# Column norms of q and k from one broadcast product, in a fused attention and two-layer kernel on one core

## The chip, the core and the metric

One core of a Trainium2 chip runs the whole program. TensorE (PE) multiplies matrices and loads its weights ahead of them (PEld), VectorE (DVE) and ScalarE (ACT) work on tiles in SBUF and PSUM, GpSimd (POOL) and SyncE (SP) mostly issue transfers. Each engine runs its own instructions in their order, and semaphores join them. The metric is the time of one execution on the device, in microseconds; less is better. The times are medians of several runs.

## What is computed

The inputs q, k and v are 6016 x 256. Each column of q and k is divided by its norm, and the softmax runs over the 256 columns of q for each column of k:

```python
qn = q / (np.linalg.norm(q, axis=1, keepdims=True) + 1e-06)
kn = k / (np.linalg.norm(k, axis=1, keepdims=True) + 1e-06)
s = kn.transpose(0, 2, 1) @ qn / tau
s = s - s.max(-1, keepdims=True)
a = np.exp(s)
a /= a.sum(-1, keepdims=True) + 1e-09
x = v @ a                                   # 6016 x 256
h = x @ w_in                                # 256 -> 2048
x2 = (s1 * np.maximum(h, 0) ** 2 + b) @ w_out
h2 = x2 @ w_in2
out = (np.maximum(h2, 0) + alpha * np.minimum(h2, 0)) @ w_out2
```

## The kernel before

The kernel never forms v @ a. It folds the 256 x 256 matrix a into the first layer's weights (a @ w_in, eight blocks w1_block) and then treats both layers alike: 12 runs (6 pairs of token tiles for each layer) of 8 steps, each step with seven 512-column products on x and four on g, and each product in three passes over halves hi and lo of its operands. That main part starts near 56 us and goes to the end.

The change lies ahead of it, from about 40 to 56 us. Until 40 us the rows of q and k come in by 16 chunks (CHUNKS). ScalarE squares them into sq, VectorE adds the squares into sq_sum, and TensorE builds k^T q (scores, into s_acc) chunk by chunk. It does so in two halves, m = 0 and m = 1, of 128 columns of k each (the partitions of s_acc). For the last six chunks (late onward) the second half is put off, so that the first half is whole early. Then comes a chain over four engines:

- TensorE sums the squares over the partitions into cols_ps, a column of four numbers for each partition: 128 columns of q twice, 128 of k twice.
- ScalarE takes the root. VectorE refines it with one Newton step (reciprocal, times the sum, plus the root, halved, plus 1e-6) and inverts it, four columns wide (rnorm).
- The norms of q are needed along the free dimension. So VectorE writes them on a diagonal (rq_diag), TensorE multiplies that with ones, and ScalarE copies the product out (rq_row).
- For each half m: largest(m) on VectorE makes the logits, their maximum and its negative. soften(m) on ScalarE takes Exp and its sum. turn_a(m) on TensorE transposes, and a_copy(m) on ScalarE copies that half of a to SBUF. inverse_sum(m) on VectorE gives the scale for w1_copy.

Between these, in fixed places, stands the preparation of the first two token tiles. turn_v(0, t, b) turns a square-blocked tile of v on VectorE (two instructions for each t). x_high(0, i) on ScalarE writes the hi half of operand i, x_low(0, i) on VectorE the lo half, and x_sums makes the four sums of tiles. The operands come in the order X_ORDER: i = 0 and 1 are the first tile's blocks and need two turns, i = 2 is a block of the second tile and needs all four:

```python
sc.wait_ge(v_turned, 2 * CB * run + (2, 2, 4)[min(i, 2)])
```

w1_block(0) and (1) need the first half of a, w1_block(2) and (3) the second (a_copied); behind them TensorE starts step 0. The order on each engine is written out by hand. link(...) makes VectorE wait for its own instruction before the next one.

Of the kernel before, what the change touches and what calls it, by code (L numbers as in the profile page):

```python
# [5 lines left out]
ACT = mybir.ActivationFunctionType  # L6
ALU = mybir.AluOpType
# [79 lines left out]
def build(nc, q, k, v, tau, moe_w_in, moe_w_out, moe_s, moe_b, moe2_w_in, moe2_w_out, moe2_alpha, out):  # L87
# [17 lines left out]
    with ExitStack() as ctx:  # L105
# [49 lines left out]
        rq_row = at("rq_row", 170 * K, [C], F32)  # L155
        rq_diag = at("rq_diag", 171 * K, [CB, P], F32)
# [3 lines left out]
        root = col[:, 4:8]  # L160
        rroot = col[:, 8:12]
        ratio = col[:, 12:16]
        twice = col[:, 16:20]
        norm = col[:, 20:24]
        rnorm = col[:, 24:28]
# [23 lines left out]
        cols_ps = acc[1][:, 0, 0:16]  # L189
        scal_ps = h_d[:, 16:20]  # L190
        alpha_ps = h_d[:, 32:32 + NF]
        rq_ps = acc[1][:, 1, 0:C]
# [18 lines left out]
        diag_ready = sem("diag_ready")  # L211
        rq_ready = sem("rq_ready")
        rq_copied = sem("rq_copied")
# [269 lines left out]
        def _(pe):  # L483
# [139 lines left out]
            for a in range(2):  # L623
                for b in range(CB):
                    mm = pe.matmul(cols_ps[:, 2 * a + b:2 * a + b + 1], sq_sum[:, a, 0, b * P:(b + 1) * P],
                                   ones[:, 0:1], start=True, stop=True)
            mm.then_inc(cols_ready, 1)
            scores(late, 1)
            scores(late + 1, 1, range(CHUNK // 2))
            pe.wait_ge(diag_ready, 1)  # L630
            for b in range(CB):
                mm = pe.matmul(rq_ps[:, b * P:(b + 1) * P], ones[:], rq_diag[:, b, :], start=True, stop=True)
            mm.then_inc(rq_ready, 1)
            scores(late + 1, 1, range(CHUNK // 2, CHUNK))
# [30 lines left out]
        def _(sc):  # L665
# [231 lines left out]
        def _(ve):  # L897
# [224 lines left out]
            ve.wait_ge(root_ready, 1)  # L1122
# [85 lines left out]
```

## Time and profile before

| | |
|---|---|
| median of 3 runs | 1035.77 us (1034.98 to 1036.99) |
| the profiled execution | 1035.88 us |
| its span, first to last instruction | 1034.1 us |
| TensorE busy | 1027.3 us, 99% of the span |
| VectorE busy | 847.0 us, 82% |
| ScalarE busy | 617.2 us, 60% |
| GpSimd busy | 59.4 us, 6% |
| granted TensorE clock, mean | 1.000 |

The span runs from the first instruction to the last; the execution takes 1.8 us more. An engine's busy time counts its instructions and not its waits for others. All starts below are in us from the start of the span, and all rows come from this one execution.

### The profile page before, as it was taken

What the parts mean: (1) busy time and instruction counts of PE and PEld (TensorE: products, weight loads), DVE (VectorE), ACT (ScalarE), POOL (GpSimd) and SP (SyncE); (2) the same over time, 40 slices, a digit from 0 to 9 for tenths busy, and PEclk for the clock granted to TensorE, in tenths of its full rate; (3) what the DMA queues carried; (4) which work ended last, traced back from release to release, by engine and by line L of the source; (5) the groups of instructions that cost most, each with busy time, mean ns of one, the idle gap of its engine ahead of it and who ended that gap; (6) DMA issues with size and microseconds to landing.
All of it is one profiled execution on the core that took longest, in us unless ns stands there. A gap on an engine that the chain in (4) does not pass through costs nothing.

```text
span 1034.1 us, 13282 instructions
## 1 busy us (share of the span) xinstructions
PE 1027.3 (99%) x4579; PEld 857.2 (83%) x4579; DVE 847.0 (82%) x1287; ACT 617.2 (60%) x1031; POOL 59.4 (6%) x88
## 2 busy tenths in 40 slices
PE   9999999999999999999999999999999999999998
PEld 7768888888888888888998888888888888888997
DVE  6888888888888888788998888777768777877875
ACT  6577776666567566666776675455545455455543
POOL 1023000000000000000661000000000000000000
PEclk9999999999999999999999999999999999999999
DMA  9853303202402311300741606004104203200201
GB/s 356 265 87 60 62 1 130 55 1 83 102 1 81 83 17 53 108 1 31 246 148 56 237 1 176 9 0 157 27 1 143 41 1 124 42 1 0 41 1 36
DMA packets 130851, 79.26 MB, mean 77 GB/s; under 512 B 98450, under 2 KB 107232, under 8 KB 130784
## 3 DMA queue, kind: packets, MB, share of 16 engines
q1 hardware_dynamic: 125536, 71.63, 23.2%
q0 software_dynamic: 4096, 6.44, 2.9%
q8 instruction: 36, 0.59, 0.3%
q10 hardware_dynamic: 1152, 0.34, 0.1%
q14 instruction: 31, 0.25, 0.1%
HBM read 50.54 MB, written 27.72 MB: 76 GB/s over the span
## 4 chain that ended last, share of the span: by engine, by line
PE 94%; DVE 2%; DMA 1%; SPq 1%; ACT 0%; issue 0%; DVEq 0%; ACTq 0%
PE acc L487 16%; PE acc L486 16%; PE acc L485 16%; PE hab L485 8%; PE hab L486 8%; PE hab L487 8%; PE hcd L487 6%; PE hcd L486 6%; PE hcd L485 6%; DMA qk_raw<-in_q_dram 1%; DVE sq_sum L1117 1%; SPq L329 1%; PE acc L601 1%; DVE xf L929 0%; ACT sq L843 0%
## 5 line engine op out<-in xcount | busy, mean ns | idle before, releaser
L767 ACT ACTIVATE g_hi<-cb 128x512 fp32r<-128x512 f32 (+1 forms) x384 | 233.8, 620 | 196.6 <-DVE cb L999 123.5
L487 PE MATMUL acc<-g_hi,wo_lo 128*128 128x512 f32 (+1 forms) x766 | 295.2, 385 | 0.0
L485 PE MATMUL acc<-g_hi,wo_hi 128*128 128x512 f32 (+1 forms) x766 | 295.2, 385 | 0.0
L486 PE MATMUL acc<-g_lo,wo_hi 128*128 128x512 f32 (+1 forms) x766 | 295.1, 385 | 0.0
L1005 DVE TENSOR_TENSOR g_lo<-cb,g_hi 128x512 fp32r<-128x512 f32 (+1 forms) x384 | 246.6, 683 | 41.3 <-ACT g_hi L767 39.2
L486 PEld LDWEIGHTS acc<-g_lo,wo_hi 128*128 128x128 f32 x766 | 143.8, 188 | 27.1
L485 PEld LDWEIGHTS acc<-g_hi,wo_hi 128*128 128x128 f32 x766 | 143.8, 188 | 27.0
L487 PEld LDWEIGHTS acc<-g_hi,wo_lo 128*128 128x128 f32 x766 | 143.8, 188 | 26.9
L999 DVE SCALAR_TENSOR_TENSOR cb<-cb,alph 128x512 f32<-128x512 f32 (+1 forms) x192 | 142.2, 741 | 21.0 <-ACT cb L737 14.9
L485 PE MATMUL hab<-x_hi,ws_hi 128*128 128x512 f32 (+1 forms) x384 | 149.7, 390 | 0.0
L486 PE MATMUL hab<-x_lo,ws_hi 128*128 128x512 f32 (+1 forms) x384 | 148.0, 385 | 0.0
L487 PE MATMUL hab<-x_hi,ws_lo 128*128 128x512 f32 (+1 forms) x384 | 148.0, 385 | 0.0
L987 DVE SCALAR_TENSOR_TENSOR cb<-hcd,sign,u 128x512 f32<-128x512 f32 (+1 forms) x96 | 70.5, 734 | 51.6 <-issue 51.6
L485 PE MATMUL hcd<-x_hi,ws_hi 128*128 128x512 f32 (+1 forms) x288 | 111.0, 385 | 0.0
L487 PE MATMUL hcd<-x_hi,ws_lo 128*128 128x512 f32 (+1 forms) x288 | 110.9, 385 | 0.0
L486 PE MATMUL hcd<-x_lo,ws_hi 128*128 128x512 f32 (+1 forms) x288 | 110.9, 385 | 0.0
L995 DVE SCALAR_TENSOR_TENSOR cb<-cb 128x512 f32<-128x512 f32 (+1 forms) x140 | 95.8, 685 | 4.8
L984 DVE TENSOR_TENSOR cb<-hcd,u 128x512 f32<-128x512 f32 (+1 forms) x96 | 65.0, 677 | 37.8 <-issue 22.9
L737 ACT ACTIVATE u<-hab,sign 128x512 f32<-128x512 f32 (+1 forms) x96 | 64.6, 673 | 51.3 <-PE hab L487 51.2
L737 ACT ACTIVATE u<-hab 128x512 f32<-128x512 f32 (+1 forms) x96 | 56.3, 586 | 58.5 <-PE hab L487 58.4
L485 PEld LDWEIGHTS hab<-x_hi,ws_hi 128*128 128x128 f32 x384 | 72.1, 188 | 16.8 <-ACT u L737 1.9
L486 PEld LDWEIGHTS hab<-x_lo,ws_hi 128*128 128x128 f32 x384 | 72.1, 188 | 13.8 <-issue 0.7
(130 smaller groups left out, 968.5 us busy)
## 6 DMA issues: line engine op xcount, KB each, us to landing
x_dram<-x_hi SPq DMA_DIRECT2D x35, 256.0 KB, 2.2
x_dram<-x_lo SPq DMA_DIRECT2D x35, 256.0 KB, 2.6
x_hi<-x_dram SPq DMA_DIRECT2D x35, 256.0 KB, 5.0
x_lo<-x_dram SPq DMA_DIRECT2D x35, 256.0 KB, 5.3
out_dram<-y_sq SPq DMA_DIRECT2D x40, 128.0 KB, 2.9
v_raw<-in_v_dram SPq DMA_DIRECT2D x36, 128.0 KB, 3.4
qk_raw<-in_k_dram SPq DMA_DIRECT2D x8, 512.0 KB, 11.3
qk_raw<-in_q_dram SPq DMA_DIRECT2D x8, 512.0 KB, 12.1
```

Of the source, the lines that this page charges most:

```text
L329: sp.dma_start(qk_raw[:, slot, a, 0:r, :], chunk_rows(x, i))\
L485: pe.matmul(dst, w_hi, m_hi, start=start, stop=False, skip_group_check=True)
L486: pe.matmul(dst, w_hi, m_lo, start=False, stop=False, skip_group_check=True)
L487: return pe.matmul(dst, w_lo, m_hi, start=False, stop=stop, skip_group_check=True)
L601: mm = pe.matmul(w1_banks[i], a_t[:, b, m * P:(m + 1) * P], win[:, 2 * h + g, b, :], start=(b == 0), stop=(b == CB - 1))
L737: sc.activation(dst[:, 0:w], h_a[n % 2][:, 0:w], ACT.Copy, scale=scale).then_inc(done, 1)
L767: sc.activation(g_hi[:, blk, 0:w], cb[:, blk, 0:w], ACT.Copy).then_inc(g_hi_done[blk], 1)
L984: ve.tensor_tensor(out_, bank[:, 0:w], part[:, 0:w], ALU.add).then_inc(sum_done[blk], 1)
L987: ve.scalar_tensor_tensor(out=out_, in0=bank[:, 0:w], scalar=sign[:, f:f + 1], in1=part[:, 0:w], op0=ALU.mult, op1=ALU.add).then_inc(sum_d ...
L995: ve.scalar_tensor_tensor(out=c, in0=c, scalar=0.0, in1=c, op0=ALU.max, op1=ALU.mult)\
L999: ve.scalar_tensor_tensor(out=c, in0=c, scalar=alph[:, f:f + 1], in1=c, op0=ALU.mult, op1=ALU.max)\
L1005: ve.tensor_tensor(g_lo[:, blk, 0:w], cb[:, blk, 0:w], f32(g_hi[:, blk, 0:w]), ALU.subtract)\
```

## The change

The sums of q's squares are no longer made as a column. One product with ones as the weights puts the sum of each of the 256 columns of q on every partition, along the free dimension, and k's two columns stand behind it: cols_ps is 258 wide. Root, Newton step and reciprocal run over all 258 columns (root and rnorm are tiles of their own now), so that rnorm's first 256 columns are what rq_row was; the diagonal, its product and the copy are gone. On VectorE the small copies of scale and alpha come ahead of the root, both turns of the first tile come behind the first logits, and the second logits come ahead of the first two x_low and of the second tile's turns. On ScalarE x_high(0, 0) and (0, 1) come behind a_copy(0), and soften(1) ahead of x_high(0, 2). On TensorE the scores of the second half run on until one row of chunk 14 is done, and then comes turn_a(0).

```diff
-        cols_ps = acc[1][:, 0, 0:16]
+        cols_ps = acc[1][:, 0, 0:C + CB]
...
             pe.wait_ge(squares_added, ADDED[-1] + 1)
-            for a in range(2):
-                for b in range(CB):
-                    mm = pe.matmul(cols_ps[:, 2 * a + b:2 * a + b + 1], sq_sum[:, a, 0, b * P:(b + 1) * P],
-                                   ones[:, 0:1], start=True, stop=True)
+            pe.matmul(cols_ps[:, 0:C], ones[:], sq_sum[:, 0, 0, :], start=True, stop=True)
+            for b in range(CB):
+                mm = pe.matmul(cols_ps[:, C + b:C + b + 1], sq_sum[:, 1, 0, b * P:(b + 1) * P], ones[:, 0:1],
+                               start=True, stop=True)
             mm.then_inc(cols_ready, 1)
-            scores(late, 1)
-            scores(late + 1, 1, range(CHUNK // 2))
-            pe.wait_ge(diag_ready, 1)
-            for b in range(CB):
-                mm = pe.matmul(rq_ps[:, b * P:(b + 1) * P], ones[:], rq_diag[:, b, :], start=True, stop=True)
-            mm.then_inc(rq_ready, 1)
-            scores(late + 1, 1, range(CHUNK // 2, CHUNK))
-            for i in range(late + 2, CHUNKS - 2):
+            for i in range(late, CHUNKS - 2):
                 scores(i, 1)
+            scores(CHUNKS - 2, 1, range(1))
             turn_a(0)
-            for i in range(CHUNKS - 2, CHUNKS):
-                scores(i, 1)
+            scores(CHUNKS - 2, 1, range(1, ROWS_OF[CHUNKS - 2]))
+            scores(CHUNKS - 1, 1)
...
-            sc.activation(root, cols_ps[:, 0:4], ACT.Sqrt, bias=tiny).then_inc(root_ready, 1)
+            sc.activation(root[:], cols_ps, ACT.Sqrt, bias=tiny).then_inc(root_ready, 1)
             sc.activation(unused[:, 1:2], ones[:, 0:1], ACT.Exp)
-            sc.wait_ge(rq_ready, 1)
-            sc.activation(rq_row[:], rq_ps, ACT.Copy).then_inc(rq_copied, 1)
-            x_high(0, 0)
-            x_high(0, 1)
...
             soften(0)
             a_copy(0)
+            x_high(0, 0)
+            x_high(0, 1)
+            soften(1)
             x_high(0, 2)
-            soften(1)
             w1_copy(0)
...
-            link(ve.reciprocal(rroot, root))
-            link(ve.tensor_tensor(ratio, cols_ps[:, 0:4], rroot, ALU.mult))
-            link(ve.tensor_tensor(twice, ratio, root, ALU.add))
-            link(ve.tensor_scalar(norm, twice, 0.5, 1e-6, ALU.mult, ALU.add))
-            link(ve.reciprocal(rnorm, norm))
-            for b in range(CB):
-                last = ve.tensor_scalar(rq_diag[:, b, :], ident[:], rnorm[:, b:b + 1], None, ALU.mult)
-            last.then_inc(diag_ready, 1)
...
+            ve.wait_ge(root_ready, 1)
+            link(ve.reciprocal(rnorm[:], root[:]))
+            link(ve.tensor_tensor(rnorm[:], cols_ps, rnorm[:], ALU.mult))
+            link(ve.tensor_tensor(rnorm[:], rnorm[:], root[:], ALU.add))
+            link(ve.tensor_scalar(rnorm[:], rnorm[:], 0.5, 1e-6, ALU.mult, ALU.add))
+            link(ve.reciprocal(rnorm[:], rnorm[:]))
+            link(ve.tensor_scalar(rk, rnorm[:, C:C + CB], rtau, None, ALU.mult))
...
-                                             in1=rq_row[:], op0=ALU.mult, op1=ALU.mult))
+                                             in1=rnorm[:, 0:C], op0=ALU.mult, op1=ALU.mult))
...
-            ve.wait_ge(rq_copied, 1)
             largest(0)
-            x_low(0, 0, x_hi_done, x_split)
+            for b in range(CB):
+                turn_v(0, 0, b)
             inverse_sum(0)
-            x_low(0, 1, x_hi_done, x_split)
...
+            largest(1)
+            for i in range(2):
+                x_low(0, i, x_hi_done, x_split)
             for b in range(CB):
                 turn_v(0, 1, b)
-            largest(1)
             x_sums(0)
             inverse_sum(1)
```

The order of the instructions, at the places of which the prediction speaks. First ScalarE from the root on, before the change (prob is the Exp of soften, a_t the copy of a_copy, w_tmp<-hab the first w1_copy, ws_hi<-w_tmp w0_high):

```order
L846 ACTIVATE col<-acc,col 128x4 [waits cols_ready,consts_ready]
...
L855 ACTIVATE prob,col<-logit,col 128x256 [waits nmax_ready]
L860 ACTIVATE a_t<-acc 128x2x128 [waits a_turned]
L693 ACTIVATE x_hi_55<-xf 128x512 [waits v_turned]
L855 ACTIVATE prob,col<-logit,col 128x256 [waits nmax_ready]
L670 ACTIVATE w_tmp<-hab,col 128x4x128 [waits w1_ready,rsum_ready]
L679 ACTIVATE ws_hi<-w_tmp 128x128 [waits w1_copied]
L860 ACTIVATE a_t<-acc 128x2x128 [waits a_turned]
```

And the same place after it:

```order
L831 ACTIVATE root<-acc,col 128x258 [waits cols_ready,consts_ready]
...
L836 ACTIVATE prob,col<-logit,col 128x256 [waits nmax_ready]
L841 ACTIVATE a_t<-acc 128x2x128 [waits a_turned]
L678 ACTIVATE x_hi_55<-xf 128x512 [waits v_turned,consts_ready]
L678 ACTIVATE x_hi_55<-xf 128x512 [waits v_turned]
L836 ACTIVATE prob,col<-logit,col 128x256 [waits nmax_ready]
L678 ACTIVATE x_hi_55<-xf 128x512 [waits v_turned]
L655 ACTIVATE w_tmp<-hab,col 128x4x128 [waits w1_ready,rsum_ready]
L664 ACTIVATE ws_hi<-w_tmp 128x128 [waits w1_copied]
L841 ACTIVATE a_t<-acc 128x2x128 [waits a_turned]
```

The third x_high, the one that waits for four turns, stood ahead of the second Exp and stands behind it now; ahead of the second a_t copy it stands in both. The first two x_high moved behind the first a_t copy.

VectorE from the first logits to the sums of tiles, before the change (v_raw is the first tile of v, v_first the second):

```order
L1140 SCALAR_TENSOR_TENSOR logit<-acc,col,rq_row 128x256 [waits s_done,rq_copied]
L1142 TENSOR_REDUCE col<-logit 128x1 [waits dve_chain]
L1143 TENSOR_SCALAR col<-col 128x1 [waits dve_chain]
L953 TENSOR_TENSOR x_lo_57<-xf,x_hi_55 128x512 [waits x_hi_done]
...
L953 TENSOR_TENSOR x_lo_57<-xf,x_hi_55 128x512 [waits x_hi_done]
...
L929 STREAM_TRANSPOSE xf<-v_first 128x512 [waits v_first_loaded,dve_chain]
L929 STREAM_TRANSPOSE xf<-v_first 128x512 [waits v_first_loaded]
L1140 SCALAR_TENSOR_TENSOR logit<-acc,col,rq_row 128x256 [waits s_done]
...
L934 TENSOR_TENSOR xf<-xf 128x512 [waits v_turned]
```

And after it, from the norm chain on:

```order
L1114 RECIPROCAL rnorm<-root 128x258 [waits root_ready,dve_chain]
...
L1118 RECIPROCAL rnorm<-rnorm 128x258 [waits dve_chain]
L1119 TENSOR_SCALAR col<-rnorm,col 128x2 [waits dve_chain]
L1123 SCALAR_TENSOR_TENSOR logit<-acc,col,rnorm 128x256 [waits s_done,dve_chain]
...
L912 STREAM_TRANSPOSE xf<-v_raw 128x512 [waits v_loaded] x2
...
L1123 SCALAR_TENSOR_TENSOR logit<-acc,col,rnorm 128x256 [waits s_done]
...
L936 TENSOR_TENSOR x_lo_57<-xf,x_hi_55 128x512 [waits x_hi_done] x2
L912 STREAM_TRANSPOSE xf<-v_first 128x512 [waits v_first_loaded] x2
L917 TENSOR_TENSOR xf<-xf 128x512 [waits v_turned]
```

The second logits passed two x_low and the two turns of v_first, and nothing of VectorE's work stands between those turns and the sums of tiles any longer.

TensorE from the norms' products to the first block of weights, before the change (qk_raw are the scores, ident,prob a turn):

```order
L625 MATMUL acc<-ones,sq_sum 128x1 [waits squares_added]
L625 MATMUL acc<-ones,sq_sum 128x1 x3
...
L632 MATMUL acc<-rq_diag,ones 128x128 [waits diag_ready]
L632 MATMUL acc<-rq_diag,ones 128x128
...
L590 MATMUL acc<-ident,prob 128x128 [waits exp_done]
L590 MATMUL acc<-ident,prob 128x128
L579 MATMUL acc<-qk_raw 128x256 [waits qk_loaded0]
L579 MATMUL acc<-qk_raw 128x256
L579 MATMUL acc<-qk_raw 128x256 [waits qk_loaded1]
L601 MATMUL hab<-win,a_t 128x512 [waits a_copied,win_loaded0]
```

And after it:

```order
L614 MATMUL acc<-sq_sum,ones 128x256 [waits squares_added]
L616 MATMUL acc<-ones,sq_sum 128x1 x2
...
L570 MATMUL acc<-qk_raw 128x256 [waits qk_loaded0]
L581 MATMUL acc<-ident,prob 128x128 [waits exp_done]
L581 MATMUL acc<-ident,prob 128x128
L570 MATMUL acc<-qk_raw 128x256 [waits qk_loaded0]
L570 MATMUL acc<-qk_raw 128x256 [waits qk_loaded1]
L592 MATMUL hab<-win,a_t 128x512 [waits a_copied,win_loaded0]
```

The two products with the diagonal are gone from between the scores, and one row of scores moved from behind the first turn to ahead of it: 13 rows stand ahead of it now, where 12 did, and two behind it, where three did.

## Rows read from the trace of the kernel before

**Rows 1.** Busy time of each engine by stretch: stretch, length, then by engine, clock, DMA.

```profile
36.00:60.00 24.00, 23.52 (x94) 15.79 (x93) 20.11 (x50) 14.38 (x30) 2.49 (x2) 1.00 0.80 165
...
150.00:500.00 350.00, 350.00 (x1560) 292.55 (x1559) 297.73 (x465) 220.45 (x388) 8.05 (x13) 1.00 0.20 61
```

**Rows 2.** Waits of TensorE's matmul queue from 56 us on: in total, times, longest.

```profile
PE hab L660 <- ACT y_raw L884: 0.2, 1, 0.2
```

**Rows 3.** Timeline, TensorE and its weight loads: start, length, what, idle time before.

```profile
40.75 0.97 PEld L625 LDWEIGHTS acc<-ones,sq_sum 128*128 128x128 f32 x8 [0.74 <-DVE sq_sum L1120]
...
41.63 2.46 PEld L579 LDWEIGHTS acc<-qk_raw 128*128 128x128 f32 x12
...
47.36 0.20 PEld L590 LDWEIGHTS acc<-ident,prob 128*128 128x128 f32 x2 [0.22 <-ACT prob L855]
...
47.64 1.46 PE L579 MATMUL acc<-qk_raw 128*128 128x256 f32 x6
...
51.81 0.20 PEld L590 LDWEIGHTS acc<-ident,prob 128*128 128x128 f32 x2 [0.97 <-ACT prob L855]
...
53.00 0.30 PEld L601 LDWEIGHTS acc<-win,a_t 128*128 128x128 f32 x2 [0.72 <-ACT a_t L860]
53.00 3.70 PE L601 MATMUL acc<-win,a_t 128*128 128x512 f32 x8
```

**Rows 4.** Timeline, ScalarE.

```profile
41.90 0.26 ACT L846 ACTIVATE col<-acc,col 128x4 f32<-128x4 f32 x1 [3.33 <-PE acc L625]
...
50.15 0.63 ACT L693 ACTIVATE x_hi<-xf 128x512 fp32r<-128x512 f32 x1 [1.93 <-DVE xf L929]
...
51.16 0.51 ACT L855 ACTIVATE prob<-logit,col 128x256 f32<-128x256 f32 x1 [0.38 <-DVE col L1143]
...
51.67 0.67 ACT L670 ACTIVATE w_tmp<-hab,col 128x512 f32<-128x512 f32 x1
...
52.37 0.31 ACT L679 ACTIVATE ws_hi<-w_tmp 128x128 fp32r<-128x128 f32 x1
...
52.58 0.37 ACT L860 ACTIVATE a_t<-acc 128x256 f32<-128x256 f32 x1
...
53.94 1.15 ACT L693 ACTIVATE x_hi<-xf 128x512 fp32r<-128x512 f32 x2
```

**Rows 5.** Timeline, VectorE.

```profile
42.20 0.18 DVE L1123 RECIPROCAL col<-col 128x4 f32<-128x4 f32 x1 [1.50 <-ACT col L846]
...
48.20 0.17 DVE L1155 COPY alph<-hcd 128x16 f32<-128x16 f32 x1
...
48.81 1.30 DVE L929 STREAM_TRANSPOSE xf<-v_first 128x512 f32<-128x512 f32 x2
...
50.04 0.44 DVE L1140 SCALAR_TENSOR_TENSOR logit<-acc,col,rq_row 128x256 f32<-128x256 f32 x1
...
51.04 0.68 DVE L934 TENSOR_TENSOR xf<-xf 128x512 f32<-128x512 f32 x1
...
54.02 1.89 DVE L953 TENSOR_TENSOR x_lo<-xf,x_hi 128x512 fp32r<-128x512 f32 x3
```

**Rows 6.** VectorE until 61 us, grouped by form: count, busy us, mean ns of one.

```profile
L1129 DVE TENSOR_SCALAR rq_diag<-ident,col 128x128 f32<-128x128 f32 x2 | 0.5, 284 | 0.0
L965 DVE TENSOR_TENSOR ws_lo<-w_tmp,ws_hi 128x256 fp32r<-128x256 f32 x1 | 0.4, 414 | 0.0
L1148 DVE RECIPROCAL col<-col 128x1 f32<-128x1 f32 x2 | 0.3, 164 | 0.1
...
L1147 DVE TENSOR_SCALAR col<-col 128x1 f32<-128x1 f32 x2 | 0.3, 149 | 0.2 <-ACT prob L855 0.2
...
L1134 DVE TENSOR_SCALAR col<-col 128x2 f32<-128x2 f32 x1 | 0.2, 228 | 0.0
...
L1127 DVE RECIPROCAL col<-col 128x4 f32<-128x4 f32 x1 | 0.2, 178 | 0.0
...
L1126 DVE TENSOR_SCALAR col<-col 128x4 f32<-128x4 f32 x1 | 0.2, 170 | 0.0
```

More of the change, by code:

```diff
@@ L154, in build @@
         prob = at("prob", 168 * K, [CB, C], F32)
-        rq_row = at("rq_row", 170 * K, [C], F32)
-        rq_diag = at("rq_diag", 171 * K, [CB, P], F32)
+        root = at("root", 166 * K, [C + CB], F32)
+        rnorm = at("rnorm", 170 * K, [C + CB], F32)
         alpha_row = at("alpha_row", 172 * K, [P], F32)
         scal_row = at("scal_row", 172 * K + 512, [4], F32)
[L160 to L165, printed above, removed]
         scal = col[:, 28:31]
@@ L188, in build @@
         s_acc = acc[0]
-        cols_ps = acc[1][:, 0, 0:16]
+        cols_ps = acc[1][:, 0, 0:C + CB]
         scal_ps = h_d[:, 16:20]
         alpha_ps = h_d[:, 32:32 + NF]
-        rq_ps = acc[1][:, 1, 0:C]
         a_t_ps = [acc[1][:, m, 0:C].rearrange("p (b c) -> p b c", b=CB) for m in range(CB)]
@@ L210, in build @@
         root_ready = sem("root_ready")
-        diag_ready = sem("diag_ready")
-        rq_ready = sem("rq_ready")
-        rq_copied = sem("rq_copied")
         nmax_ready = sem("nmax_ready")
@@ L1120, in _ @@
             ve.tensor_tensor(sq_sum[:, :, 0, :], sq_sum[:, :, 0, :], sq_sum[:, :, 1, :], ALU.add).then_inc(squares_added, 1)
-            ve.wait_ge(root_ready, 1)
-            link(ve.reciprocal(rroot, root))
-            link(ve.tensor_tensor(ratio, cols_ps[:, 0:4], rroot, ALU.mult))
-            link(ve.tensor_tensor(twice, ratio, root, ALU.add))
-            link(ve.tensor_scalar(norm, twice, 0.5, 1e-6, ALU.mult, ALU.add))
-            link(ve.reciprocal(rnorm, norm))
-            for b in range(CB):
-                last = ve.tensor_scalar(rq_diag[:, b, :], ident[:], rnorm[:, b:b + 1], None, ALU.mult)
-            last.then_inc(diag_ready, 1)
             ve.wait_ge(cols_ready, 1)
@@ L1133, in _ @@
             link(ve.reciprocal(rtau, scal[:, 0:1]))
-            link(ve.tensor_scalar(rk, rnorm[:, 2:4], rtau, None, ALU.mult))
-            for b in range(CB):
-                turn_v(0, 0, b)
+            link(ve.tensor_copy(alph[:], alpha_ps))
+            link(ve.tensor_scalar(sign[:], alph[:], 1.0, -2.0, ALU.is_gt, ALU.mult))
+            link(ve.tensor_scalar(sign[:], sign[:], 1.0, None, ALU.add))
+            ve.wait_ge(root_ready, 1)
[5 more added lines that the diff above has]
+            link(ve.tensor_scalar(rk, rnorm[:, C:C + CB], rtau, None, ALU.mult))
             def largest(m):
@@ L1148, in inverse_sum @@
                 ve.reciprocal(rsum[:, m:m + 1], sum_eps[:, m:m + 1]).then_inc(rsum_ready, 1)
-            ve.wait_ge(rq_copied, 1)
             largest(0)
-            x_low(0, 0, x_hi_done, x_split)
+            for b in range(CB):
+                turn_v(0, 0, b)
             inverse_sum(0)
-            x_low(0, 1, x_hi_done, x_split)
-            link(ve.tensor_copy(alph[:], alpha_ps))
-            link(ve.tensor_scalar(sign[:], alph[:], 1.0, -2.0, ALU.is_gt, ALU.mult))
-            link(ve.tensor_scalar(sign[:], sign[:], 1.0, None, ALU.add))
+            largest(1)
+            for i in range(2):
+                x_low(0, i, x_hi_done, x_split)
             for b in range(CB):
                 turn_v(0, 1, b)
-            largest(1)
             x_sums(0)
```

## The prediction

> **What bounds the kernel now.** I read the stretches first [rows 1]. From 150 to 500 us TensorE is busy 350.00 us of 350, and in the stage that the change touches, 36 to 60 us, it is busy 23.52 of 24, at the full 2.4 GHz level (granted clock 1.00) in both. Then the waits of TensorE's matmul queue from 56 us to the end [rows 2]: 0.2 us in all, at the very end. So behind the first step nothing has slack to swallow a delay or to give back a gain: whatever moves the start of the first projection products moves the end by as much. The question is only when, around 53 us, TensorE gets what it waits for. The timeline answers that [rows 3]: its weight loads sat 0.22 us before the first turn of the probabilities (47.36), 0.97 us before the second (51.81), and 0.72 us at 53.00, for ScalarE's copy L860 of the second half of A. The eight passes that start there (3.70 us) feed all that follows, so the stage ends with that copy, a_copy(1), at 52.58 [rows 4]. What led to the copy: ScalarE stood still until 50.15, when VectorE had turned the second tile (L929, 48.81 plus 1.30 = 50.11) [rows 5], split that tile (x_high(0, 2)), then waited until 51.16 for the second logits, and went through prob, w1_copy(0) and w0_high(0).
>
> **The change, part by part.** Call L the start of the second logits (largest(1)), 50.04 now [rows 5].
>
> 1. Where the tile's turn goes. VectorE now runs largest(1), then x_low twice, then the two turns of v_first. ScalarE runs soften(1), then x_high(0, 2), then w1_copy(0), w0_high(0), a_copy(1); x_high(0, 2) still waits for four turns. So the copy on which TensorE waits hangs behind the turns, which hang behind the logits and the splits. From rows: the instruction behind the logits began 1.00 us after them (50.04 to 51.04), an x_low takes 0.605 from start to start (three end in 1.89, of which the last 0.68), the pair of turns 1.30, and ScalarE starts 0.04 later [rows 4, 5]: L + 1.00 + 1.21 + 1.30 + 0.04 = L + 3.55. Then x_high 0.57 (two in 1.15), w1_copy 0.70 (51.67 to 52.37), w0_high 0.21 (52.37 to 52.58): a_copy(1) starts at L + 5.03. Against 52.58 the shift is **L - 47.55**. VectorE's own sums begin at about L + 3.55 instead of 51.04, nearly the same shift, so the parts behind keep their relative places. The change gains only if the second logits start before 47.55, that is 2.49 us earlier than now.
>
> 2. What TensorE allows. The products for the norms keep their length, I take it: four 128x1 matmuls, eight passes, were 40.75 to 41.63; now two passes over 256 columns at the 0.205 us of a score pass (12 loads in 2.46) and four small ones at 0.11, 0.85 against 0.88 [rows 3]. The scores then run without a break, 13 rows of two passes: 41.63 + 26 x 0.205 = 46.96 for the first turn at the earliest. Behind that turn now six passes remain until the scores end: 47.36 to 47.64 + 1.46 = 49.10, 1.74 us. With four passes it is 1.74 - 0.41 = 1.33. So s_done(2) is at 48.29 at best, and L at least 48.33: **a loss of 0.78 us even if VectorE cost nothing.** What is saved (two products with the diagonal, the copy to rq_row, two products with ident on VectorE) is in this number already.
>
> 3. What the longer norm chain costs. ScalarE's root over 258 columns lies between the 0.37 of a PSUM copy of 256 and the 0.51 of an Exp of 256; I take 0.43 [rows 4]: 41.90 + 0.43 = 42.33, VectorE starts at 42.37. Scale, alpha and sign now fill its wait for the root: five short instructions of 0.15 to 0.17 with gaps, about 1.0 us, inside an idle time of 1.50 before L1123 [rows 5]; costed at nothing, and 1.0 if the cover were gone. Then six linked instructions with 0.035 between them [rows 6]:
> - two TENSOR_TENSOR over 258: 0.42 each, next to 0.414 for 256;
> - one TENSOR_SCALAR over 258: 170 ns for 4 columns, and from 2 to 128 columns its kind rises 56 ns (L1134, L1129), 0.44 ns a column: 0.28. At a full nanosecond it would be 0.43;
> - rk as before, 0.23;
> - **two RECIPROCAL over 258 columns, r each.** The trace has them only at 1 column (164 ns) and at 4 (178). That slope is 14 ns on 3 columns, 4.7 to 5 ns a column: r = 0.178 + 254 x 0.0049 = 1.43. The lower bound reads the 14 ns as a fixed step: TENSOR_SCALAR too rises from 149 at one column to 170 at four, though it surely costs under 1 ns a column. Then r is that of its neighbours, 0.42. The upper bound takes the shortest instruction (149) as the fixed part: 29 ns on 4 columns, 7.25 each, r = 2.02.
> I take 1.43, since it is the one reading that uses nothing but RECIPROCAL's own rows.
>
> The sum: 2 x 1.43 + 0.84 + 0.28 + 0.23 + 6 x 0.035 = 4.42, so largest(0) starts at 46.79. From logits to Exp it is 1.12 (50.04 to 51.16), from Exp to the turn 0.65 (51.16 to 51.81): first turn at 48.56, 1.6 us after TensorE was free for it. Plus 1.33: s_done(2) at 49.89, L = 49.93. Shift 49.93 - 47.55 = **+2.4 us**. Every further 0.1 us of r adds 0.2; below r = 0.63 TensorE's own order decides and the shift stays at 0.78.
>
> The Trainium skill, VectorE: DVE Perf Modes, "First, the fixed hardware budget", says that Reciprocal is an iterative divide with a repeat count of 8. If that is eight cycles a column at the page's 0.96 GHz, an estimate of r from it is 2.3 and of the shift 4.1; the rows' 4.9 ns are nearer to five cycles, and no row here is wide enough to decide.
>
> The profiled execution took 1035.88 us for a span of 1034.1, and stands 0.11 above the median of 1035.77. The shift is put on the median: 1035.77 + 2.4 = 1038.2. The measurement can hardly tell less than 0.2%, 2.1 us, from no change.
>
> **The rivals.**
> - *Cheap reciprocals* (r about 0.42). For it: the step of TENSOR_SCALAR [rows 6]. Against it: RECIPROCAL's own slope. L = 48.33, +0.8 us, 1036.6, within 0.2%. Chance 0.24.
> - *Dearer ones* (6 to 8 ns a column): r 1.8 to 2.0 and more, L 50.7 to 51.1 and beyond, +3.1 to +3.6, about 1039.2. For it: a fixed part common to all short instructions. Chance 0.24.
> - *The clock falls.* TensorE would stand 1.6 us before the first turn, and about 3.1 us (52.25 to L + 5.45) before the copy of the second half, where 0.97 and 0.72 were the longest gaps at full clock [rows 1, 3]. If the eight passes after it ran at 1.2 GHz, twice their 3.70 us, that adds 3.7: +6.1, 1041.9. Against it: no stretch of this trace shows the lower level at all. Chance 0.06.
> - *Faster.* The one way I see is that the split x_high(0, 2) does not hold up the copy of A: if the first turn and the scores came so early that L fell below 47.55. With L = 47.0 it would be -0.5 us. It needs 1.3 us fewer passes than the order has. Chance 0.04. That the later turn is absorbed somewhere behind is part of it, and [rows 2] speaks against.
>
> **How the numbers follow.** The forecast (r near 1.43) has 0.42, with its own range of +1.7 to +3.1; about two thirds of it lie above 2.1 us. Slower by over 0.2%: 0.28 + 0.24 + 0.06 = 0.58; within 0.2%: 0.14 + 0.24 = 0.38; faster 0.04. The range reaches down to the cheap case with half a microsecond of scatter, 1036.2, and up past the upper bound of r, 1040.0; outside are the clock, the gain, and a tail of each.
>
> **What would show it.** Right: RECIPROCAL over 258 columns at 1.4 us in the new trace; a gap of 1.6 us in TensorE before the first turn; ScalarE idle ahead of x_high(0, 2) until the turns of v_first end near 53.5; a_copy(1) near 55.0, and everything behind it late by the same amount, to the end. Wrong: a reciprocal near 0.42 (the loss shrinks to 0.8), or a_copy(1) before 52.6 (then part 1 is false), or the same lateness at 55 us and none at 150 (then something behind has slack that I didn't see).

## The result, and the profile after

The changed kernel takes **1038.90 us** (median, 1038.67 to 1039.12), the kernel before 1035.26 in the same comparison (1034.98 to 1036.99, eight runs each): a ratio of 1.003, interval 1.0022 to 1.0039. The change made the kernel slower by about 3.6 us by the medians, and by 2.3 to 4.0 us by the interval. The profiled execution took 1039.01 us for a span of 1037.2, where before it was 1035.88 and 1034.1.

The page of the changed kernel, its first line and busy times:

```profile
span 1037.2 us, 13266 instructions
...
PE 1025.2 (99%) x4573; PEld 856.9 (83%) x4573; DVE 850.5 (82%) x1285; ACT 616.8 (59%) x1030; POOL 60.3 (6%) x88
```

The same two stretches as in [rows 1], busy time by engine, then clock and DMA:

```profile
36.00:60.00 24.00, 20.04 (x81) 13.91 (x79) 21.57 (x42) 12.00 (x23) 2.49 (x2) 1.00 0.82 168
...
150.00:500.00 350.00, 350.00 (x1559) 292.30 (x1557) 296.08 (x463) 221.18 (x388) 5.54 (x9) 1.00 0.20 60
```

Behind the first step nothing changed: TensorE is busy 350.00 us of 350 again. Nearly all of the loss lies in the 24 us of the stage (0.31 us more appears at 59 to 64 us, see the account below), where TensorE is busy 20.04 us instead of 23.52, at an unchanged clock of 1.00. Its timeline and that of its weight loads (start, length, what, idle time before), beside [rows 3]:

```profile
41.22 0.30 PEld L614 LDWEIGHTS acc<-sq_sum,ones 128*128 128x128 f32 x2 [0.64 <-DVE sq_sum L1103]
...
42.09 5.48 PEld L570 LDWEIGHTS acc<-qk_raw 128*128 128x128 f32 x26
...
49.87 0.20 PEld L581 LDWEIGHTS acc<-ident,prob 128*128 128x128 f32 x2 [2.29 <-ACT prob L836]
...
56.65 0.30 PEld L592 LDWEIGHTS acc<-win,a_t 128*128 128x128 f32 x2 [2.65 <-ACT a_t L841]
56.65 3.70 PE L592 MATMUL acc<-win,a_t 128*128 128x512 f32 x8 [1.83 <-ACT a_t L841]
...
59.33 0.19 PEld L592 LDWEIGHTS acc<-win,a_t 128*128 128x128 f32 x1 [0.24 <-issue]
...
61.60 1.88 PE L592 MATMUL acc<-win,a_t 128*128 128x512 f32 x4
```

Where the loads idled 0.22, 0.97 and 0.72 us, two long gaps stand now: 2.29 us before the first turn of the probabilities, and 2.65 us before the products with the second half of A, which start at 56.65 instead of 53.00. (The last row is a group of four passes at full clock, and the row before it the last weight load of the eight passes; both are for comparison further down.)

ScalarE's timeline, beside [rows 4]:

```profile
42.36 0.48 ACT L831 ACTIVATE root<-acc,col 128x258 f32<-128x258 f32 x1 [3.32 <-PE acc L616]
...
52.37 0.51 ACT L836 ACTIVATE prob<-logit,col 128x256 f32<-128x256 f32 x1 [0.61 <-DVE col L1126]
...
54.78 0.63 ACT L678 ACTIVATE x_hi<-xf 128x512 fp32r<-128x512 f32 x1 [1.81 <-DVE xf L912]
55.32 0.67 ACT L655 ACTIVATE w_tmp<-hab,col 128x512 f32<-128x512 f32 x1
...
56.24 0.36 ACT L841 ACTIVATE a_t<-acc 128x256 f32<-128x256 f32 x1
...
60.76 0.69 ACT L655 ACTIVATE w_tmp<-acc,col 128x512 f32<-128x512 f32 x1 [1.00 <-PE acc L592]
```

x_high(0, 2), at 54.78, waited 1.81 us for VectorE's turns of the tile, and the copy that releases TensorE, a_copy(1), follows at 56.24. VectorE, beside [rows 5]:

```profile
40.48 0.69 DVE L1103 TENSOR_TENSOR sq_sum<-sq_sum 128x512 f32<-128x512 f32 x1
...
42.94 1.77 DVE L1114 RECIPROCAL rnorm<-root 128x258 f32<-128x258 f32 x1 [0.87 <-ACT root L831]
...
45.66 0.30 DVE L1117 TENSOR_SCALAR rnorm<-rnorm 128x258 f32<-128x258 f32 x1
45.99 1.77 DVE L1118 RECIPROCAL rnorm<-rnorm 128x258 f32<-128x258 f32 x1
48.06 0.48 DVE L1123 SCALAR_TENSOR_TENSOR logit<-acc,col,rnorm 128x256 f32<-128x256 f32 x1
...
51.21 0.48 DVE L1123 SCALAR_TENSOR_TENSOR logit<-acc,col,rnorm 128x256 f32<-128x256 f32 x1 [0.59 <-PE acc L570]
...
52.25 1.28 DVE L936 TENSOR_TENSOR x_lo<-xf,x_hi 128x512 fp32r<-128x512 f32 x2
53.45 1.30 DVE L912 STREAM_TRANSPOSE xf<-v_first 128x512 f32<-128x512 f32 x2
```

Two reciprocals of 1.77 us stand in the norm chain, and behind the second logits (51.21) come two splits and the two turns before the tile is ready. That the delay then stays whole is seen on one instruction 156 us later. Before, ScalarE's timeline has

```profile
212.29 0.60 ACT L737 ACTIVATE s<-hab 128x512 f32<-128x512 f32 x1
```

and in the changed kernel

```profile
216.26 0.60 ACT L722 ACTIVATE s<-hab 128x512 f32<-128x512 f32 x1
```

3.97 us later. The same 3.97 holds from about 62 to 515 us, about 3.81 until 970, and 3.11 at the end of this pair of executions.

One thing must be taken off before kernels are compared. The last addition of squares, which nothing in the change touches, starts at 40.00 before and 40.48 here; over all kernels of this study it lies anywhere between 39.98 and 40.80, from one profiled execution to the next. Below, **net** is how much later than before a kernel's copy of near 212 us (the one above) starts, less how much later its addition starts: here 3.97 - 0.48 = **+3.49**.

### The profile page after: what moved, and what is told of

Read it like the earlier page. It is cut to its first block, busy times and chain, and to the rows that moved or that the text cites. A ratio compares the mean times of both kernels' runs of the same rounds, so it can differ in the third digit from the quotient of the medians.

```text
span 1037.2 us, 13266 instructions
## 1 busy us (share of the span) xinstructions
PE 1025.2 (99%) x4573; PEld 856.9 (83%) x4573; DVE 850.5 (82%) x1285; ACT 616.8 (59%) x1030; POOL 60.3 (6%) x88
## 4 chain that ended last, share of the span: by engine, by line
PE 94%; DVE 2%; DMA 1%; SPq 1%; ACT 1%; issue 0%; DVEq 0%; ACTq 0%
PE acc L478 16%; PE acc L476 16%; PE acc L477 16%; PE hab L476 8%; PE hab L477 8%; PE hab L478 8%; PE hcd L476 6%; PE hcd L478 6%; PE hcd L477 6%; DMA qk_raw<-in_q_dram 1%; DVE sq_sum L1100 1%; SPq L320 1%; PE acc L592 1%; ACT sq L828 0%; DVE rnorm L1118 0%
```

## The experiments

Theory A is the prediction's mechanism: TensorE waits for a_copy(1), which hangs behind the turns of the second tile, which hang behind the second logits (start L), which hang behind the norm chain (the two wide reciprocals above all) or, if that were short, behind TensorE's own row of scores. The rivals in what follows are the clock, a cost of the order that the sum leaves out, and slack behind the stage.

| kernel | last addition | L | a_copy(1) | net | median, us | ratio (interval) |
|---|---|---|---|---|---|---|
| before | 40.00 | 50.04 | 52.58 | 0 | 1035.26 | 1 |
| changed | 40.48 | 51.21 | 56.24 | +3.49 | 1038.90 | 1.003 (1.0022 to 1.0039) |
| e1: norms alone | 39.98 | 53.94 | 57.87 | +5.84 | 1040.79 | 1.0047 (1.0035 to 1.006) |
| e2: orders alone | 40.40 | 49.49 | 54.52 | +1.57 | 1037.47 | 1.0016 (1.0007 to 1.0025) |
| e3: split behind the copy | 40.80 | 51.54 | 54.33 | +4.72 | 1040.48 | 1.0038 (1.0025 to 1.0052) |
| e4: one reciprocal | 40.41 | 49.04 | 54.07 | +1.41 | 1037.14 | 1.0013 (1.0004 to 1.0022) |
| e5: before, small copies early | 40.19 | 49.46 | 52.07 | -0.58 | 1034.94 | 0.999 (0.9981 to 0.9999) |
| e6: changed, with the probe | 39.98 | 50.72 | 55.75 | +3.51 | 1038.76 | one run |
| e8: changed, turns ahead | 40.10 | 51.37 | 54.43 | +2.24 | 1038.67 | 1.0018 (1.0009 to 1.0027) |
| e9: e2, turns ahead | 40.02 | 49.16 | 52.22 | +0.04 | 1036.15 | 0.9998 (0.9989 to 1.0007) |

Each ratio is against the kernel before in the same comparison (medians 1035.26 to 1036.12). Single executions of one kernel scatter by 1 to 4 us and the medians by a few tenths, so the fine comparisons go by the traces, one for each kernel. How well net repeats is seen on e6, which is the changed kernel with a probe far ahead of this stage: +3.51 against +3.49.

**e1, the new norms with the old orders.** The diagonal and its products are replaced as in the change; TensorE's, ScalarE's and VectorE's orders are those of before. Its core, against the changed kernel:

```diff
             # ScalarE
+            x_high(0, 0)
+            x_high(0, 1)
             soften(0)
             a_copy(0)
-            x_high(0, 0)
-            x_high(0, 1)
+            x_high(0, 2)
             soften(1)
-            x_high(0, 2)
...
             # VectorE
-            largest(0)
             for b in range(CB):
                 turn_v(0, 0, b)
+            largest(0)
+            x_low(0, 0, x_hi_done, x_split)
             inverse_sum(0)
-            largest(1)
-            for i in range(2):
-                x_low(0, i, x_hi_done, x_split)
+            x_low(0, 1, x_hi_done, x_split)
...
             for b in range(CB):
                 turn_v(0, 1, b)
+            largest(1)
```

> The wide norm chain of the changed kernel (one product with ones, root and two reciprocals over 258 columns), with all orders of the kernel before: turns of the first tile ahead of the first logits, x_low and the small copies and the second tile's turns ahead of the second logits, x_high(0,0) and (0,1) ahead of the first Exp. Times of a_copy(1) are counted from VectorE's last addition of squares (40.00 before, 40.48 after), where before stands at 12.58 and the changed kernel at 15.76, that is +3.18. Theory A (VectorE's chain through the two wide reciprocals is what makes it late, in either order): rk ends as in the changed kernel, at +7.54, the turns take 1.22 more, and from the first logits to a_copy(1) it is 7.09 as before: 15.9, +3.3 us against before, no better than the changed kernel. Theory B (the order costs, the norms don't, since the diagonal and its copy are gone): within 0.5 us of before.

Measured: net +5.84 us, some 2.5 more than the +3.3 of Theory A. Most of the difference is the clock. TensorE's timeline:

```profile
50.65 0.69 PE L581 MATMUL acc<-ident,prob 128*128 128x128 f32 x2 [3.60 <-ACT prob L835]
51.13 2.77 PE L570 MATMUL acc<-qk_raw 128*128 128x256 f32 x6
53.69 3.07 PE L592 MATMUL hab<-win,a_t 128*128 128x512 f32 x4
```

and two stretches of it (busy time by engine, then clock):

```profile
48.00:52.00 4.00, 1.35 (x5) 1.18 (x6) 3.67 (x12) 2.02 (x5) 1.27 (x1) 0.66 0.33 118
52.00:56.00 4.00, 4.00 (x8) 2.35 (x7) 3.43 (x8) 1.23 (x3) 0.00 (x0) 0.50 0.71 105
```

TensorE stood 3.60 us (its loads 4.00). The granted clock fell to 0.50, the 1.2 GHz level, while it still stood (0.62 in the microsecond from 49 to 50) and was full again from 56 on. Six score passes took 2.77 us, against 1.46 in [rows 3], and four passes of the first weight block 3.07, against 1.88 for such a group of four in the changed kernel. So TensorE lost 1.3 + 1.2 = 2.5 us, but not all of that was waited for. These two instructions show what was, the second logits on VectorE and w1_copy(0) on ScalarE:

```profile
53.94 0.48 DVE L1119 SCALAR_TENSOR_TENSOR logit<-acc,col,rnorm 128x256 f32<-128x256 f32 x1 [0.43 <-PE acc L570]
```

```profile
56.85 0.69 ACT L654 ACTIVATE w_tmp<-hab,col 128x512 f32<-128x512 f32 x1 [1.16 <-PE hab L592]
```

An estimate from the rows: with the clock held, the logits would have followed the turns (52.20 + 1.23 = 53.43) and a_copy(1) would have stood 2.54 us behind them, as in the kernel before, at 55.97; it stood at 57.87. The clock cost 1.9 us there. Without it a_copy(1), counted from the addition, is 3.4 us later than before, near the 3.3 of Theory A. Of what is left between 3.4 + 1.9 = 5.3 and 5.84, 0.3 us is the delay behind w1_copy(3) that the last section describes; 0.2 us is not explained. So the clock rival, which the changed kernel itself escapes (1.00 in every microsecond from 47 to 69), is real and near.

**e2, the old norms with the new orders.** The other half. All orders of the change are in it, the early place of the small copies and ScalarE's order too; TensorE's and the second logits' are these:

```diff
             # TensorE, against the kernel before
+            scores(CHUNKS - 2, 1, range(1))
             turn_a(0)
-            for i in range(CHUNKS - 2, CHUNKS):
-                scores(i, 1)
+            scores(CHUNKS - 2, 1, range(1, ROWS_OF[CHUNKS - 2]))
+            scores(CHUNKS - 1, 1)
...
             # VectorE
+            largest(1)
+            for i in range(2):
+                x_low(0, i, x_hi_done, x_split)
             for b in range(CB):
                 turn_v(0, 1, b)
-            largest(1)
```

> All orders of the changed kernel with the norm chain of before (four columns, diagonal, its product, rq_row). Theory A: TensorE's scores set the second logits. 13 rows and the two products with the diagonal end 0.55 later than the scores alone, so the first turn is at about 47.5, the scores end at 48.83, L is 48.87, and a_copy(1) is at L + 5.03 = 53.9, +1.3 us against before: the order alone is a loss as well, since the copy of the second half hangs behind the second tile's turns. Theory B (the order costs everything): +3 us or more. Theory C (the order is a gain that the wide norms hide): below before, -0.5 us or more.

Measured: net +1.57, and 1037.47 us. VectorE's second logits:

```profile
49.49 0.48 DVE L1142 SCALAR_TENSOR_TENSOR logit<-acc,col,rq_row 128x256 f32<-128x256 f32 x1 [1.07 <-PE acc L579]
```

and ScalarE:

```profile
53.06 0.63 ACT L694 ACTIVATE x_hi<-xf 128x512 fp32r<-128x512 f32 x1 [1.81 <-DVE xf L930]
...
54.52 0.37 ACT L859 ACTIVATE a_t<-acc 128x256 f32<-128x256 f32 x1
```

The logits come 0.55 us earlier than before and the copy 1.94 later, 5.03 us behind them. With cheap norms too, the new order loses: L must fall below 47.55 for it to pay, and TensorE's scores (1.07 us of waiting) don't allow it.

**e4, one reciprocal.** The Newton step and the second reciprocal are left out:

```diff
             link(ve.reciprocal(rnorm[:], root[:]))
-            link(ve.tensor_tensor(rnorm[:], cols_ps, rnorm[:], ALU.mult))
-            link(ve.tensor_tensor(rnorm[:], rnorm[:], root[:], ALU.add))
-            link(ve.tensor_scalar(rnorm[:], rnorm[:], 0.5, 1e-6, ALU.mult, ALU.add))
-            link(ve.reciprocal(rnorm[:], rnorm[:]))
```

> The changed kernel without the Newton step and its second reciprocal: rnorm is the plain reciprocal of the root, four instructions of VectorE fewer (0.43 + 0.43 + 0.30 + 1.77 and their gaps, 3.07 us). It leaves out the refinement and the 1e-6. Theory A: the chain is then shorter than TensorE's row of scores, so the first turn comes when 13 rows are through (26 passes from 42.09: 47.57), the scores end at 48.9, L is 49.0, a_copy(1) at 54.0: +1.0 us against before, 2.2 us better than the changed kernel and not 3.1. Theory B (everything of the chain counts): 3.1 us better, +0.1 against before.

Measured: net +1.41, 2.08 us less than the changed kernel, though 3.05 us of VectorE's chain were taken out. Its weight loads and its second logits:

```profile
47.54 0.36 PEld L581 LDWEIGHTS acc<-ident,prob 128*128 128x128 f32 x2
```

```profile
49.04 0.48 DVE L1119 SCALAR_TENSOR_TENSOR logit<-acc,col,rnorm 128x256 f32<-128x256 f32 x1 [1.53 <-PE acc L570]
```

The first turn follows the scores with no idle time before it, and VectorE waits 1.53 us for the second half's scores. The bound has passed to TensorE's row, at +1.08 us by a_copy(1) less the addition (54.07 - 40.41 = 13.66, before 12.58). This is the prediction's "loss even if VectorE cost nothing", there put at 0.78.

**e6, the reciprocal's price by width.** Ahead of everything on VectorE, one tile of ones is inverted over seven widths:

```diff
+            link(ve.memset(flat_in, 1.0))
+            for wd in (1, 2, 4, 16, 64, 128, 512):
+                link(ve.reciprocal(flat_out[:, 0:wd], flat_in[:, 0:wd]))
```

> The changed kernel with seven reciprocals more at the very start of VectorE's work, on a tile of ones, 1, 2, 4, 16, 64, 128 and 512 columns wide. Only their durations count. The 258 columns took 1766 ns. Theory A (a constant price a column on a fixed part): 6.23 ns a column above the 164 ns of one, so 0.26, 0.56, 0.96 and 3.35 us at 16, 64, 128 and 512. Theory B (the price falls as the width grows, as 4.7 ns between 1 and 4 columns might be read, or rises by blocks): other values at 16 to 128 with the same 1766 at 258. The kernel itself starts its squares later by up to some us.

VectorE grouped by form (count, busy us, mean ns of one):

```profile
L1097 DVE RECIPROCAL prob<-logit 128x512 f32<-128x512 f32 x1 | 3.4, 3354 | 0.0
L1097 DVE RECIPROCAL prob<-logit 128x128 f32<-128x128 f32 x1 | 1.0, 953 | 0.0
L1097 DVE RECIPROCAL prob<-logit 128x64 f32<-128x64 f32 x1 | 0.6, 554 | 0.0
L1097 DVE RECIPROCAL prob<-logit 128x16 f32<-128x16 f32 x1 | 0.3, 253 | 0.0
L1097 DVE RECIPROCAL prob<-logit 128x4 f32<-128x4 f32 x1 | 0.2, 178 | 0.0
L1097 DVE RECIPROCAL prob<-logit 128x2 f32<-128x2 f32 x1 | 0.2, 166 | 0.0
L1097 DVE RECIPROCAL prob<-logit 128x1 f32<-128x1 f32 x1 | 0.2, 164 | 0.0
```

From 2 columns on the line is straight: (3354 - 953) / 384 = 6.25 ns a column, (253 - 178) / 12 = 6.25 again, and (178 - 166) / 2 = 6, with 153 ns fixed. 153 + 258 x 6.25 = 1766 ns, which is what the chain shows. Only the single column lies off the line, at 164 ns where the line has 159. So from 1 to 4 columns the time rises by only 14 ns, 4.7 a column: one of the two widths that the trace of before had misleads. The probe itself cost nothing (net +3.51, the changed kernel's own).

**e3, the split behind the copy.** In the changed kernel x_high(0, 2) goes behind a_copy(1):

```diff
             # ScalarE
-            x_high(0, 2)
...
             a_copy(1)
+            x_high(0, 2)
```

> The changed kernel with one move on ScalarE: x_high(0, 2) behind a_copy(1) instead of ahead of w1_copy(0). Theory A: a_copy(1) comes 2.2 us sooner (near 54.0 where the changed kernel has 56.24), but VectorE's work behind the second tile's turns is not sooner; its last merge of step 0 cannot begin before 60.7 where it began at 61.48, so only 0.8 us comes back at the end: +2.4 us against before. Theory B (a_copy(1) alone decides): 2.2 us come back, +1.0 to +1.4.

Measured: a_copy(1) started at 54.33 and no longer waits for the turns, yet the kernel got slower, net +4.72. Its weight loads and matmuls:

```profile
58.30 0.19 PEld L476 LDWEIGHTS hab<-x_hi,ws_hi 128*128 128x128 f32 x1 [0.55 <-ACT w_tmp L655]
...
61.11 0.19 PEld L476 LDWEIGHTS hcd<-x_hi,ws_hi 128*128 128x128 f32 x1 [2.27 <-DVE x_lo L936]
...
61.92 3.08 PE L592 MATMUL acc<-win,a_t 128*128 128x512 f32 x4
```

its stretches:

```profile
60.00:64.00 4.00, 2.86 (x7) 1.48 (x8) 3.34 (x10) 2.41 (x5) 1.20 (x1) 0.81 0.66 94
64.00:68.00 4.00, 4.00 (x13) 2.40 (x11) 2.77 (x5) 1.70 (x3) 1.20 (x1) 0.77 0.40 60
```

The wait moved by one product: TensorE had the copy early, and then stood 2.27 us for the same tile's lower part. Counted from the addition, the product that waited started no sooner than in the changed kernel (61.11 - 40.80 = 20.31; there 60.78 - 40.48 = 20.30). Up to here Theory A holds, and the last merge of step 0 also came 0.89 us sooner (L899 at 61.56, in the changed kernel at 62.13, both less the addition), near the 0.8 us that it names. What it did not foresee is the clock. The granted clock fell behind this gap (0.73, 0.50, 0.50 and 0.56 in the four microseconds from 62 to 66), and the four passes that take 1.88 us at full clock took 3.08. Of five runs four took 1040.09 to 1040.96 and one 1038.04. If that one kept its clock, the edit alone is worth some 0.9 us against the changed kernel, again the size that Theory A gives it; only one run was profiled, so that is not shown.

**e8 and e9, the second tile's turns ahead of the second logits.** In the changed kernel (e8) and in e2 (e9) only this moves:

```diff
             # VectorE
             inverse_sum(0)
+            for b in range(CB):
+                turn_v(0, 1, b)
             largest(1)
             for i in range(2):
                 x_low(0, i, x_hi_done, x_split)
-            for b in range(CB):
-                turn_v(0, 1, b)
```

> The changed kernel with one move on VectorE: the two turns of the second tile ahead of the second logits, everything else as it is. VectorE stood still 0.59 us before those logits, so the turns (1.25) make them 0.65 later, 51.86, but ScalarE's x_high(0, 2) need not wait any more: Exp at 52.98, x_high 53.55, w1_copy(0), w0_high(0), and a_copy(1) at 55.1 where it was 56.24; VectorE's sums begin at 54.1 where they began at 54.78. Theory A (what hangs behind the second tile's turns is late): 0.7 to 1.1 us better than the changed kernel, +2.5 to +2.9 against before. Theory B (the second logits decide, the later they are the worse): 0.6 us worse, +4.2. If TensorE's clock falls in the gaps, some us more than either.

> The norm chain of before with the orders of the changed kernel, but the second tile's turns ahead of the second logits. With the changed order alone it was +1.57 us counted from the last addition of squares (a_copy(1) 54.52, sums from 53.06). Theory A: the turns fill VectorE's idle 1.07 us before the second logits, which start at 49.67; a_copy(1) at 52.8 and the sums at 51.9, so 1.2 to 1.6 us come back: +0.0 to +0.4 against before. Theory B (the place of the turns isn't what costs in the order): +1.3 to +1.8 as it was.

VectorE of e8:

```profile
50.16 1.28 DVE L912 STREAM_TRANSPOSE xf<-v_first 128x512 f32<-128x512 f32 x2
51.37 0.44 DVE L1123 SCALAR_TENSOR_TENSOR logit<-acc,col,rnorm 128x256 f32<-128x256 f32 x1
```

and its copy on ScalarE:

```profile
54.43 0.37 ACT L841 ACTIVATE a_t<-acc 128x256 f32<-128x256 f32 x1
```

The logits of e8 stand 11.27 us behind the addition, against 10.73 in the changed kernel, so the turns cost them 0.54; but the copy now stands 3.06 us behind the logits instead of 5.03. Net +2.24, 1.25 us better than the changed kernel (by the ratios, 1.003 and 1.0018, about as much, though their intervals overlap). In e9 the same move takes +1.57 to +0.04, no difference from before (0.9998). So most of what the new orders lose hangs on one thing, the turns behind the logits.

It is not all. e9 holds the early small copies as well, which alone gain 0.58 us (e5, next); if such gains add, its other moves still cost about 0.6. TensorE's weight loads in e9 show where:

```profile
57.35 0.19 PEld L485 LDWEIGHTS hcd<-x_hi,ws_hi 128*128 128x128 f32 x1 [0.75 <-DVE x_lo L954]
```

a_copy(1) is 0.38 us earlier than before, counted from the addition (52.22 - 40.02 = 12.20 against 12.58), but two x_low now stand between the logits and the sums of tiles, and TensorE waits 0.75 us for the next x_low; there the 0.38 is lost again. e8 has the same wait of 0.75 us. What e8 loses against e9 (2.24 - 0.04 = 2.20 us), with the same orders in both, is the price of the wide norms.

**e5, the kernel before with one part of the change.** Only scale, alpha and sign move ahead of the wait for the root:

```diff
+            ve.wait_ge(cols_ready, 1)
+            link(ve.tensor_copy(scal, scal_ps[:, 0:3]))
+            link(ve.reciprocal(rtau, scal[:, 0:1]))
+            link(ve.tensor_copy(alph[:], alpha_ps))
+            link(ve.tensor_scalar(sign[:], alph[:], 1.0, -2.0, ALU.is_gt, ALU.mult))
+            link(ve.tensor_scalar(sign[:], sign[:], 1.0, None, ALU.add))
             ve.wait_ge(root_ready, 1)
...
-            ve.wait_ge(cols_ready, 1)
-            link(ve.tensor_copy(scal, scal_ps[:, 0:3]))
-            link(ve.reciprocal(rtau, scal[:, 0:1]))
...
-            link(ve.tensor_copy(alph[:], alpha_ps))
-            link(ve.tensor_scalar(sign[:], alph[:], 1.0, -2.0, ALU.is_gt, ALU.mult))
-            link(ve.tensor_scalar(sign[:], sign[:], 1.0, None, ALU.add))
```

> The kernel before with one move on VectorE: the five short instructions for scale, alpha and sign (0.15 to 0.17 each, about 0.98 us with gaps) go into its wait of 1.50 us for the root. Theory A: the second tile's turns are 0.6 us sooner, the second logits wait for the scores (TensorE, 49.10) and start at 49.45 instead of 50.04, and the end comes 0.5 to 0.6 us sooner. Theory B: they were hidden, no change in the end, a_copy(1) where it was.

VectorE:

```profile
48.24 1.30 DVE L929 STREAM_TRANSPOSE xf<-v_first 128x512 f32<-128x512 f32 x2
49.46 0.44 DVE L1143 SCALAR_TENSOR_TENSOR logit<-acc,col,rq_row 128x256 f32<-128x256 f32 x1
```

Turns and logits start 0.57 and 0.58 us earlier than in [rows 5] (0.76 and 0.77 with the addition's 0.19 taken off), a_copy(1) follows at 52.07 instead of 52.58 (the logits follow the turns at once; Theory A had them wait for the scores), and the gain is still there at 212 us, net -0.58. The median is 1034.94 against 1035.54, ratio 0.999 (0.9981 to 0.9999). It is the one version that stands ahead of both kernels, by less than the 0.2% that the prediction named as its bound; that the gain is real rests on the trace as much as on the interval.

## Why the prediction was right, and where its size was off

The forecast was a loss of 2.4 us, to 1038.2; measured were +3.6 and 1038.90. Mechanism, place and sign held; one term of the sum was too small. That the time is only 0.7 us off, where the loss is 1.2 off, is luck: the median of the kernel before came out 0.5 us lower in the larger comparison (1035.26) than in the one that the forecast started from (1035.77).

- **What bounds the kernel.** Right. TensorE has no slack behind 56 us: the delay at 62 us is the delay at 515 us to 0.01. Only at the end does this pair of executions give back some (3.97 to 3.11).
- **Where the turns go.** Right. The prediction put a_copy(1) 5.03 us behind L; it was 56.24 - 51.21 = 5.03, and in e2 and e4 as well. The shift L - 47.55 gives 3.66, and 56.24 - 52.58 is 3.66. That it fits to the digit is partly luck: the sum up to x_high(0, 2) was 3.57 instead of 3.55, and from there on 1.46 instead of 1.48. ScalarE idled 1.81 us ahead of x_high(0, 2), as said, at 54.78 where 53.5 was forecast: 1.28 later, of which 0.48 is the later addition and 0.80 the next point.
- **The longer norm chain: the term that failed is r.** "I take 1.43" for a RECIPROCAL over 258 columns; it is 1.77. The step from 1 to 4 columns was read as a slope of 4.9 ns a column; e6 shows 6.25 from 2 columns on. (The rows' own 14 ns on 3 columns are 4.7, which gives 1.36; the slip to 4.9 brought the forecast a little nearer.) Two of them: 0.67 us. The rest of the chain was off by 0.13 in all (root 0.48 instead of 0.43, the product of alike width 0.43 and the scalar one 0.30 instead of 0.42 and 0.28, 0.10 instead of 0.04 from the root to VectorE). Together L came at 50.73 with the addition's lateness taken off, 0.80 behind the forecast's 49.93. So the rival of **dearer reciprocals** (6 to 8 ns a column, +3.1 to +3.6) describes the kernel better than the forecast case did.
- **The rule on the reciprocal.** The Trainium skill, VectorE: DVE Perf Modes, "First, the fixed hardware budget", gives Reciprocal a repeat count of 8. Read as eight cycles a column it gave the prediction's estimate of r = 2.3. The run lies between that and the forecast's 1.43, at 1.77: 6.25 ns a column, by the page's 0.96 GHz ("Specifications") an estimate of six cycles. So reading the repeat count as cycles was too high here. That a reciprocal costs several times its neighbours was right (1.77 us against 0.30 for the TENSOR_SCALAR of the same width).
- **What TensorE allows.** 0.85 us for the products: 0.87 measured (41.22 to 42.09). 26 score passes: 5.33 forecast, 5.48 measured, 0.211 each. Before the first turn 1.6 us of waiting were forecast and 2.29 measured, before the copy 3.1 and 2.65. In e4, where the chain is short, TensorE's row decides as the prediction said, at +1.08 instead of +0.78.
- **The small copies at nothing.** Right: they lie in the wait for the root, of which 0.87 us is still left, and in the kernel before the same move even gains 0.58 (e5).
- **The clock.** Rightly given little for this kernel, but for a thin reason. In the changed kernel gaps of 2.29 and 2.65 us left the clock at 1.00; 4.00 us in e1, and 2.27 us soon after others in e3, did not. The price was put at 3.7 us, for the eight passes behind the second gap; in e1 the clock fell behind the first one and cost about 1.9 (the estimate above).

The account from the trace: 2.38 forecast + 0.67 for the reciprocals + 0.13 for the rest of the chain = 3.18, the start of a_copy(1) counted from the addition (15.76 us against 12.58); + 0.31 that appears at 59 to 64 us (below) = 3.49; + 0.48 of the addition's own lateness = 3.97 in the middle of the run. Of these, 3.1 to 3.6 are left at the end. The rise from 3.18 to 3.49 and the loss at the end are measured and not explained.

The parts do not add: norms alone cost about 3.9 with the clock's 1.9 taken off, orders alone 1.57, both 3.49. In e1 the wide norms meet turns and splits that stand ahead of the logits; in the changed kernel VectorE's turns wait behind them instead. Without the clock e1 would come out some tenths later than the changed kernel. What the new orders gave the new norms, as far as these runs show, is mainly that TensorE's gaps stayed such that its clock held.

## What to carry to other kernels

Turning a narrow column computation into a wide one saves products and copies, but an elementwise operation with a high price per column is then paid over the whole width: measure that operation at two widths near the one wanted, since very short ones (1 and 4 columns here) can give the wrong slope. When two instructions are swapped in an in-order queue, write the time of the awaited result as a sum from the swapped instruction (a_copy(1) = L + 5.03), and find the L at which it pays (47.55); here that one line decided the change, and no run came near. Check the next product too: in e9, with the turns moved back, it was the two x_low behind the logits that TensorE waited for. Taking away the last wait is no gain if the next product needs the same late tile (e3), and a gap that grows by a microsecond or two may cost as much again through the clock.

## What was not expected of the hardware

- The clock falls only behind some gaps. TensorE stood 2.29 us and, later, 2.65 us (by its weight loads) and stayed at 2.4 GHz; in e1 it stood 4.00 us, and the granted clock was 0.50, the 1.2 GHz level, from 50 to 56 us; in the profiled run of e3 it stood 2.27 us up to 61, not long after other gaps, and the granted clock was 0.50 from 63 to 65 and for a part of the microseconds on either side (0.73 and 0.56). No run here shows where the line between them is.
- RECIPROCAL over 128 partitions in f32: 153 ns and 6.25 ns a column from 2 to 512 columns, 164 ns at one.
- w1_copy(3) (w_tmp<-acc, 60.76 in the changed kernel) waits for the eight passes on the second half of A. It starts 1.42 to 1.45 us behind the start of their last weight load in the kernels with the wide norms (60.76 - 59.33 = 1.43 in the changed kernel; e1, e4, e6, e8), and 1.11 to 1.12 us behind it in those with the narrow ones (before, e2, e5, e9), whatever the order; in e3 ScalarE was busy until then, so it can't be told. This is the 0.31 us of the account. What in the wide norms does it stays open; no run tried it. The two rows of before:

```profile
55.68 0.19 PEld L601 LDWEIGHTS acc<-win,a_t 128*128 128x128 f32 x1 [0.24 <-issue]
```

```profile
56.80 0.69 ACT L670 ACTIVATE w_tmp<-acc,col 128x512 f32<-128x512 f32 x1 [0.68 <-PE acc L601]
```

- Between about 975 and 1028 us six profiled executions (the changed kernel, e3, e4, e6, e8, and also e5, which has the narrow norms) win back 0.8 us on the one of the kernel before, their steps there being about 0.2 us shorter each; e2 wins back 0.2, e1 and e9 nothing. It goes with neither the norms nor the orders. That too is open.
